# TensorE's first block of the routed stage moved ahead of its wait for the plan, and two plan numbers read later in each block

## What is computed

```python
# x: (3072, 384) tokens, after the attention-like recurrence and a leaky MLP
skip_score = x @ w_skip
do_compute = skip_score > 0
out = x.copy()
xc = x[do_compute]
logits = xc @ w_gate                       # 8 experts
e_idx = np.argmax(logits, axis=1)
gate_w = probs[np.arange(len(xc)), e_idx]  # softmax of the logits
for e in range(E):
    mask = e_idx == e
    h = np.maximum(xc[mask] @ w1[e], 0.0)  # w1[e]: (384, 1024)
    y[mask] = gate_w[mask, None] * (h @ w2[e])
out[do_compute] = xc + y
```

## Time and profile before

| what | value |
|---|---|
| three runs | 720.26, 728.21, 728.44 us; median 728.21 |
| profiled execution | 721.34 us, its span 719.5 us |
| mean granted TensorE clock | 0.986 |
| TensorE busy | 686.2 us (95% of the span) |
| VectorE, ScalarE, GpSimd busy | 413.5, 306.9, 84.8 us |
| routed stage | about 550 us to the end |

### The profile page before, as it was taken

One profiled execution on the slowest core, in us unless ns is written; L12 is line 12 of the kernel. 1 busy time (PEld: TensorE's weight loads), 2 busy tenths in 40 slices (PEclk: granted clock), 3 DMA queues, 4 the chain that ended last, 5 costly groups with the idle time before them and its releaser, 6 DMA issues.

```text
span 719.5 us, 14041 instructions
## 1 busy us (share of the span) xinstructions
PE 686.2 (95%) x4361; PEld 645.4 (90%) x4362; DVE 413.5 (57%) x862; ACT 306.9 (43%) x665; POOL 84.8 (12%) x110
## 2 busy tenths in 40 slices
PE   8989999999999999999999999999997999999993
PEld 7989999999999999999999999999993778888883
DVE  8875756645656565555657555534557562655751
ACT  4535434434334443343444335333442452735550
POOL 6430000100010010001000100100101113222311
PEclk9999999999999999999999999999999899999997
DMA  8826624220422421142222222006014881462400
GB/s 248 256 87 198 198 67 133 67 64 15 129 61 66 124 75 27 45 130 65 67 68 82 59 61 86 12 18 235 12 53 160 303 310 51 149 248 84 165 20 8
DMA packets 38585, 77.43 MB, mean 108 GB/s; under 512 B 8472, under 2 KB 26806, under 8 KB 38528
## 3 DMA queue, kind: packets, MB, share of 16 engines
q1 hardware_dynamic: 33632, 62.37, 28.0%
q10 hardware_dynamic: 2432, 9.76, 3.7%
q0 software_dynamic: 2464, 4.58, 2.1%
HBM read 61.09 MB, written 12.41 MB: 102 GB/s over the span
## 4 chain that ended last, share of the span: by engine, by line
PE 87%; DVE 6%; issue 3%; ACT 2%; ACTq 0%; DVEq 0%; POOL 0%; POOLq 0%
PE bank L703 29%; PE bank L721 27%; PE bank L852 8%; PE bank L808 7%; PE bank L585 4%; PE bank L641 3%; PE bank L636 3%; PE bank L654 2%; PE bank L836 2%; PE bank L679 1%; PE bank L623 1%; DVE h_sb L1232 1%; PE bank L800 1%; ACT h_sb L947 0%; ACT w_hi L976 0%
## 5 line engine op out<-in xcount | busy, mean ns | idle before, releaser
L1232 DVE TENSOR_TENSOR h_sb<-h_sb,bank 128x384 f32<-128x384 f32 x128 | 70.9, 554 | 168.9 <-ACT h_sb L947 163.7
L947 ACT ACTIVATE h_sb<-bank 128x384 f32<-128x384 f32 x128 | 62.9, 491 | 245.1 <-PE bank L703 235.0
L703 PE MATMUL bank<-x_hi,win_hi 128*128 128x384 f32 x384 | 134.4, 350 | 2.4 <-DVE win_lo L1254 1.9
L721 PE MATMUL bank<-wout_hi,g_hi 128*128 128x394 f32 x384 | 131.5, 342 | 0.0
L721 PE MATMUL bank<-wout_hi,g_lo 128*128 128x394 f32 x384 | 131.4, 342 | 0.0
L721 PE MATMUL bank<-wout_lo,g_hi 128*128 128x394 f32 x384 | 131.3, 342 | 0.0
L703 PE MATMUL bank<-x_hi,win_lo 128*128 128x384 f32 x384 | 129.4, 337 | 0.0
L703 PE MATMUL bank<-x_lo,win_hi 128*128 128x384 f32 x384 | 129.2, 336 | 0.0
L1239 DVE TENSOR_TENSOR g_lo<-h_sb,g_hi 128x384 fp32r<-128x384 f32 x128 | 71.3, 557 | 33.4 <-ACT g_hi L954 32.2
L954 ACT ACTIVATE g_hi<-h_sb 128x384 fp32r<-128x384 f32 x128 | 66.6, 520 | 44.6 <-DVE h_sb L1232 41.3
L703 PEld LDWEIGHTS bank<-x_hi,win_hi 128*128 128x128 f32 x384 | 72.1, 188 | 8.9 <-issue 6.5
(11 more groups left out here) (207 smaller groups left out, 972.4 us busy)
## 6 DMA issues: line engine op xcount, KB each, us to landing
raw<-in_experts SPq DMA_DIRECT2D x32, 768.0 KB, 6.3
rkt<-in_rk_t SPq DMA_DIRECT2D x46, 192.0 KB
rkn<-in_rk_nat SPq DMA_DIRECT2D x21, 384.0 KB
v<-in_v_nat SPq DMA_DIRECT2D x24, 192.0 KB, 2.9
z_rows<-z_sb SPq DMA_DIRECT2D x24, 192.0 KB, 2.7
out<-z_sb SPq DMA_DIRECT2D x24, 192.0 KB, 2.9
stage<-in_win ACTq DMA_DIRECT2D x4, 768.0 KB, 4.4
stage<-in_wout_t ACTq DMA_DIRECT2D x4, 768.0 KB, 6.2
```

Source lines behind the costliest of these rows:

```text
L703: mm = pe.matmul(h_ps[t % 2][:, 0:GT], a[:, kk, cols], b[G % 2][:, kk, :], start=n == 0, stop=n == 3 * KT - 1)
L721: mm = pe.matmul(z_ps[i][:, 0:ZW], a[t % 3][:, tok], b[:, f, :], start=f == 0 and j == 0, stop=f == FT - 1 and j == 2)
L947: act.activation(h_sb[t % 2][:], h_ps[t % 2][:, 0:GT], ACT.Copy, scale=SLOPE).then_inc(s_h_scaled, 1)
L1232: dve.tensor_tensor(h_sb[t % 2][:], h_sb[t % 2][:], h_ps[t % 2][:, 0:GT], ALU.max).then_inc(s_leaky, 1)
```

## The change

On TensorE alone. Ahead of the loop, `turn_rows(0)` and `first_product(0, 0, 0)` move in front of the wait for `s_plan_done` and the load of the number of blocks; the second `turn_rows` stays behind these. In the loop a block's own expert and parity (`cur`, `odd`), which the second product needs, are loaded behind the next block's first product and no longer ahead of L836. The number of instructions is the same.

```diff
-            pe.wait_ge(s_plan_done, 1)
-            blocks = pe.value_load(plan[0:1, TOTAL:TOTAL + 1], min_val=E, max_val=BLOCKS)
             pe.wait_ge(rows_in[0], 16)
             turn_rows(0)
             pe.wait_ge(s_zt_lo, 1)
             first_product(0, 0, 0)
+            pe.wait_ge(s_plan_done, 1)
+            blocks = pe.value_load(plan[0:1, TOTAL:TOTAL + 1], min_val=E, max_val=BLOCKS)
             pe.wait_ge(rows_in[1], 16)
             turn_rows(1)
             with pe.Fori(0, (BLOCKS + 1) // UNROLL) as jj:
...
                             nxt_odd = pe.value_load(plan[0:1, bass.ds(PARITY + j + 1, 1)], min_val=0,
                                                     max_val=1)
-                            cur = pe.value_load(plan[0:1, bass.ds(EXPERT + j, 1)], min_val=0, max_val=E - 1)
-                            odd = pe.value_load(plan[0:1, bass.ds(PARITY + j, 1)], min_val=0, max_val=1)
 
                             pe.wait_ge(s_relu_done, j + 1)
...
                             with pe.If(j < blocks - 1):
                                 pe.wait_ge(s_zt_lo, j + 2)
                                 first_product((u + 1) % 2, nxt_odd * EW, PIECES * nxt)
+
+                            cur = pe.value_load(plan[0:1, bass.ds(EXPERT + j, 1)], min_val=0, max_val=E - 1)
+                            odd = pe.value_load(plan[0:1, bass.ds(PARITY + j, 1)], min_val=0, max_val=1)
 
                             with pe.If(j < blocks - 2):
```

## The result

The changed kernel's median is 715.45 us (20 runs, 710.56 to 725.03), that of the kernel before 724.79 us (20 runs, 720.26 to 733.46). The ratio is 0.987, 95% interval 0.9842 to 0.9897: 7.5 to 11.5 us faster. The profiled execution took 715.63 us (span 713.8) against 721.34 (span 719.5). Runs that fell in a disturbed state are left out of the ratio.

What follows compares the result with a forecast made beforehand. TensorE carries 87% of the chain, stalled at seams by number reads and at the entry by the plan. Loop 5.0 plus entry 0.45 is 5.45, called 5.5, off the median 728.21: 722.5 us named, range 712.5 to 728.5.

Steps and rivals of the forecast that it cites:

- The seams' 8.05 us: Between loop blocks: TensorE's stall summed over 13 seams, all removed by taking two number reads away ahead of L836.
- The relay at the entry: Routed stage's entry: first product starts near 557.3 instead of 558.24, 0.9 us earlier.
- D: Rival at the seams: L836 waits for something else that merely ends with the fourth number; chance 0.03.
- the entry: Start of routed stage: first product ends 0.45 us earlier if the clock falls as before, 3.2 if it stays up.
- the loop: All seams together: 5.10 + 0.3 − 0.4 = 5.0 us gained, bounds 8.05 and −1.2.
- the seam 6 to 7: Loop: its 0.84 us is eaten in block 7 by a gather landing behind an expert's weights; 0.1 left.
- the list of what is late next: Loop: seam gains ahead of blocks held by VectorE's chain or the gather are eaten; whole gains sum to 5.10.
- Stalls of 0.4 each in 5, 9 and 12: Loop, these blocks: 0.4 us of new stall each from the register work moved behind the first product.
- VectorE's data work: Loop: from w_lo to next zt_lo VectorE runs without pause, about 10.0 us a block against TensorE's 9.56.
- A (eaten): Rival: VectorE's work and the gathers return the seams' gain; loop gives 0 to 2 us, 726 to 728; chance 0.17.
- B: Rival: seams return 8.05 and the clock holds at the entry, 11.3 us; 717 from the median; chance 0.12.
- C (no cover): Rival: sequencer's lead behind the first product doesn't cover 1.5 us; with none, 11 us slower, 739; chance 0.04.

Runs made afterwards that it cites:

- run 2: Kernel before with only the loop part of the change, entry still waiting for the plan: ratio 0.9894 to the kernel before.
- run 3: The changed kernel measured again, nothing altered: ratio 0.9888 to the kernel before.
- run 1: Kernel before with only the entry part of the change, all four numbers still read ahead of the turned rows: ratio 0.9979 to the kernel before.
- run 9: Changed kernel with VectorE's three reads for the next block moved ahead of its wait for the turned rows: ratio 0.9813 to the kernel before.
- run 4: Changed kernel with the block's own two numbers read behind the turning of the rows instead of ahead: ratio 0.9931 to the kernel before.
- run 7: Kernel before with four more filler matmuls ahead of the wait for the plan: ratio 0.9985 to the kernel before.
- run 5: Changed kernel with ScalarE's three reads for the next block moved ahead of its wait for the first product: ratio 0.9875 to the kernel before.
- run 6: Changed kernel with ScalarE and VectorE also taking the first rows ahead of the plan wait and block-count read: ratio 0.9845 to the kernel before.
- run 10: Changed kernel with both ScalarE's and VectorE's reads for the next block moved ahead: ratio 0.9811 to the kernel before.
- run 8: Changed kernel with the two numbers read twice behind the first product: block 0 to 13 132.46 us in one execution, no ratio given.
- run 11: Changed kernel with both engines' reads moved ahead, and ScalarE and VectorE taking the first rows ahead of the plan: ratio 0.9812 to the kernel before.

## Why the prediction was right, and where not

**The mechanism held.** The seams' 8.05 us were the four reads, and all but 0.1 of it went (runs 2 and 3 too). The relay at the entry came out as worked out: the first product started 0.98 us earlier against the plan, 0.9 forecast. That L836 waits for something else, which merely ends with the fourth number (D, 0.03), is out: it started 0.06 us behind the end of the last read, at all 13 seams, and with two reads fewer ahead of L834 no seam kept more than 0.01.

**The time: 722.5 us named, 715.45 measured, inside 712.5 to 728.5.** Of the 7 us between them 3.4 come from the level: the three runs at hand had their median at 728.21, twenty have it at 724.79. The rest is the gain, which was larger than forecast. That the profiled execution took 715.63 us, where its own trace gave 715.8, is luck: its stage was 8.6 us shorter instead of 5.5, and slow stretches of the clock ahead of the plan took 2.9 back.

**The size was low: 5.5 forecast, 9.3 between the medians (7.5 to 11.5).** Three terms were mis-sized.

The first is the entry. I took 0.45 us, the case in which the clock falls again, and wrote 3.2 for the other. Both were measured, 0.39 in run 3 and 3.06 in the profiled run. The step that failed is the choice of one of them "since TensorE is still idle 2.9 us in one piece". Behind it stood one case, the fall to 0.50 after 2.34 us of idle time. But with an idle piece of 2.55 to 2.83 us there the clock held in five of eight traces. If the old entry always falls, as in its two traces, and the new one holds in five of eight, the entry is worth some 2 us. The program does not settle which: the changed kernel was at 1.00 there in its first trace and at 0.50 in run 3's. I also missed that block 0's transposes stand behind reads that wait for block 1's rows, and so need the loop's part (run 1: block 0 at plan + 8.74); in the full change this cost 0.1 us, in run 9 with the same entry 0.7.

The second is the seam 6 to 7, of which I left 0.1 of 0.84 because block 7's rows land late. After, they had landed 4.3 us behind L834 of block 7, ahead of the engine's need at 5.0, and the seam's gain was kept. The gather had been issued 1.45 us ahead of an expert's weights (632.92 and 634.37) and no longer 0.33. That this order is the reason is not shown, though most traces side with it: from the gather's issue until TensorE's sequencer has the rows it took 7.1 to 7.3 us where the weights follow by 0.3 (before, runs 1, 4, 7, 9) and 6.0 to 7.0 where they follow by 1.5 (the change, runs 2, 3, 5, 6). That the margin is thin is shown by runs 4 and 9, where the rows were 1.26 and 1.43 us late. In both the gather itself was issued later, 1.0 and 0.7 us ahead of L834 of block 7, against 1.6 to 2.6 in the others named here; why is open.

The third is the list of what is late next. It named the right blocks. Stalls of 0.4 each in 5, 9 and 12 were measured as 0.31, 0.30 and 0.63 behind the first product, and the waits for w_lo ahead of it, which I had inside "eaten", as 0.56, 0.47 and 0.71. What was wrong is the cause: I held VectorE's data work for the bound, 10.0 us a block. Run 10 shows that most of that was reading numbers, 3.7 us of 4.7 on two engines. In the sum the loop gave 5.7 against 5.0: 8.0 from the seams, less 2.7 of new stalls, and 0.4 because the eight transposes, whose weight loads now follow the second product's without a gap, take 0.76 us from first to last start instead of 0.82 (0.65 in sum), while the other groups of matmuls together run 0.3 longer.

**Adding up.** Loop 5.7 and entry 2 are 7.7 us, inside the measured interval. The 1.6 us up to the difference of the medians are not accounted for by these traces. Slow stretches of the clock early in the kernel differ from trace to trace, are not the edit's, and move the plan by up to 4 us (554.3 to 558.4 in the fourteen).

**Rivals.** A (eaten) was partly at work: 4.7 us of stalls are left over, 2.7 more than before. Both halves of B occurred in the profiled run, closed seams and a clock that held; its 11.3 less the 2.7 of new stalls is the 8.6 measured. In run 3, of the same program, the clock fell. C (no cover) is the boundary that run 8 found, at about 3 us of reads, and run 4 in another form.

## What to carry over

Where a weight load or matmul waits for "issue", look at the same moment on the engine's sequencer: here a register read of 0.75 us cost nothing while queued work ran (in ten of twelve blocks the turned rows started 0.23 us behind the first product's last start, with two reads between them as without), and its full time once the queue had run dry (two reads, 1.5 us, and 1.53 us of stall in block 7 of run 4). Put such reads where the most work is queued, and ahead of waits for transfers rather than behind them (runs 1, 4 and 11). If a chain runs through two engines that each read numbers ahead of their link, move both before judging either, and look at what the moved reads now stand in front of (run 10).

## Not expected of the hardware

The profile names the semaphore's sender as the releaser even where the waiting engine's own sequencer was the last: w_lo of run 5, "2.13 <-ACT w_hi", with w_hi's first piece done 1.8 us before. And the granted clock did not follow the same program: with an idle piece of 2.67 and 2.80 us at the same place it stayed at 1.00 in the first trace and went to 0.50 for 6.8 us in run 3's, 2.8 us of difference at the last matmul of the first product (plan + 5.98 against 8.74).
